# Weights of the second feed-forward quad split up and moved into the attention stage of a fused attention and two-MLP kernel

## The reference, cut to what matters

```python
# attention: batch 4, heads 8, seq 576, head_dim 64; factor 4
out_d = sm_attn(q_d, k_d, v_d)             # q, k, v averaged over groups of 4 tokens
mask = np.abs(pos[:, None] - pos[None, :]) < factor
scores = np.where(mask, scale * np.matmul(q, k.transpose(0, 1, 3, 2)), -1e9)
out_local = softmax(scores) @ v            # banded attention
x = np.repeat(out_d, factor, axis=2) + out_local      # -> 2304 tokens x 512
h = x @ w_in;  x = (h - np.tanh(h)) @ w_out                           # d_ff 2048
x = (1 / (1 + np.exp(-(x @ w_gate))) * (x @ w_val)) @ w_out           # d_ff 1536
```

## Time and profile before

| | |
|---|---|
| median of 3 runs | 947.53 us (947.15 to 951.25) |
| the profiled execution | 949.2 us, of it a span of 947.1 us from the first to the last instruction |
| granted TensorE clock, mean over the span | 0.971 |
| busy | PE 901.8 us (95%), DVE 577.1, ACT 387.3, POOL 300.5 |
| attention, up to the first product of quad 0 | 0 to 121.4 us |
| from there to where PE has no more gaps for a while | 121.4 to 165 us |

### The profile page before, as it was taken

One profiled execution on the slowest core, in us unless ns is written; L12 is line 12 of the kernel. 1 busy time (PEld: TensorE's weight loads), 2 busy tenths in 40 slices (PEclk: granted clock), 3 DMA queues, 4 the chain that ended last, 5 costly groups with the idle time before them and its releaser, 6 DMA issues.

```text
span 947.1 us, 15642 instructions
## 1 busy us (share of the span) xinstructions
PE 901.8 (95%) x6056; PEld 844.4 (89%) x6056; DVE 577.1 (61%) x901; ACT 387.3 (41%) x750; POOL 300.5 (32%) x251
## 2 busy tenths in 40 slices
PE   7877787999999999999998999999999999999997
PEld 5766577989999999999998999999999999999996
DVE  8777745666876566866668555556544456544445
ACT  4765645443533234433334544444322234222221
POOL 5978677674102000111015555741200001000000
PEclk8898969999999999999999999999999999999999
DMA  9677628667746464645421567679775555575411
GB/s 259 170 217 218 168 77 306 222 237 261 275 153 227 147 228 151 221 158 211 165 92 45 217 262 279 274 292 365 282 285 208 217 214 214 212 279 201 199 45 67
DMA packets 46089, 197.01 MB, mean 208 GB/s; under 512 B 3936, under 2 KB 15552, under 8 KB 33216
## 3 DMA queue, kind: packets, MB, share of 16 engines
q1 hardware_dynamic: 41984, 166.66, 48.9%
q0 software_dynamic: 4032, 29.36, 8.3%
HBM read 139.90 MB, written 56.10 MB: 207 GB/s over the span
## 4 chain that ended last, share of the span: by engine, by line
PE 79%; POOL 9%; DVE 3%; DMA 3%; issue 3%; ACT 2%; SPq 0%; POOLq 0%; DVEq 0%; ACTq 0%
PE banks L787 43%; PE banks L855 18%; PE banks L971 16%; DMA v_four<-in_v_dram 2%; POOL v_four L554 1%; POOL win L595 1%; POOL prob L561 1%; POOL mid L601 1%; POOL v_down L558 1%; ACT win L1035 1%; PE banks L765 1%; DMA qk<-in_k_dram 1%; POOL prob_d L561 1%; DVE x_op L1297 1%; PE banks L742 0%
## 5 line engine op out<-in xcount | busy, mean ns | idle before, releaser
L787 PE MATMUL banks<-x_op,pair 128*128 128x384 f32 x1512 | 278.5, 336 | 1.7 <-DVE cg_sum L1457 1.7
L787 PEld LDWEIGHTS banks<-x_op,pair 128*128 128x128 f32 x1512 | 266.7, 189 | 9.7 <-DVE cg_sum L1457 2.1
L855 PE MATMUL banks<-g_parts,mid 128*128 128x384 f32 x1152 | 228.4, 337 | 7.3 <-DVE x_all L1377 5.3
L855 PEld LDWEIGHTS banks<-g_parts,mid 128*128 128x128 f32 x1152 | 203.0, 189 | 10.2 <-DVE x_all L1377 7.3
L787 PE MATMUL banks<-x_op,win 128*128 128x384 f32 x1008 | 206.7, 342 | 4.3 <-ACT c_sum L1071 4.3
L787 PEld LDWEIGHTS banks<-x_op,win 128*128 128x128 f32 x1008 | 182.3, 193 | 5.5 <-ACT c_sum L1071 3.8
L971 PE MATMUL banks<-wout,p_parts 128*128 128x512 f32 x648 | 163.6, 393 | 1.7 <-issue 1.7
L1377 DVE TENSOR_TENSOR x_all<-banks,x_all 128x384 f32<-128x384 f32 x168 | 93.0, 555 | 83.3 <-PE banks L855 82.9
L971 PEld LDWEIGHTS banks<-wout,p_parts 128*128 128x128 f32 x648 | 120.3, 188 | 22.6 <-issue 2.1
L1482 DVE TENSOR_TENSOR x_all<-banks,x_all 128x512 f32<-128x512 f32 x90 | 62.1, 690 | 113.4 <-PE banks L971 113.4
L617 POOL DMA_DIRECT2D wout<-kept_out x12 | 6.4, 537 | 211.4 <-PE banks L971 211.4
(11 more groups left out here) (93 smaller groups left out, 1008.8 us busy)
## 6 DMA issues: line engine op xcount, KB each, us to landing
pair<-kept_pair SPq DMA_DIRECT2D x24, 1792.0 KB, 10.8
win<-kept_in SPq DMA_DIRECT2D x16, 1792.0 KB, 7.4
kept_pair<-pair SPq DMA_DIRECT2D x12, 1792.0 KB, 11.8
mid<-kept_mid POOLq DMA_DIRECT2D x16, 1024.0 KB, 5.1
kept_in<-win SPq DMA_DIRECT2D x7, 1792.0 KB, 6.8
wout<-kept_out POOLq DMA_DIRECT2D x12, 1024.0 KB, 11.7
kept_mid<-mid SPq DMA_DIRECT2D x7, 1024.0 KB, 7.0
kept_out<-wout SPq DMA_DIRECT2D x6, 1024.0 KB, 14.6
```

The source lines that it names most:

```text
L787: mm = pe.matmul(bk[:, 0:T], weights[:, w, p - 1, kk, :], x_op[:, p - 1, x, kk, :], start=(first and kk == 0 and a == 0), stop=(last and k ...
L855: mm = pe.matmul(bk[:, 0:T], w[:, wp, f, m * P:(m + 1) * P], g[:, gp, 2 * f + t, :], start=(f == 0 and a == 0), stop=(f == 1 and a == 2))
```

## The change

- GpSimd's round: `value_sums` comes last, behind `denominators` and `normalise`.
- `weight_sums(0)` is cut in two halves of two sums (rounds 2 and 3); `weight_high(0)` in two halves (ACT rounds 3 and 4); `weight_low(0)` in four quarters (GpSimd rounds 5 to 8). `plain_low(0)` is in round 9, `x_sums(0)` one sum each in rounds 11, 12, 13.
- Quad 1: `weight_sums(1)` in two halves in rounds 6 and 7, `weight_high(1)` in two halves in ACT's rounds 7 and 8, the low part on DVE (`second_weight_low`) ahead of its `first_quad(0)`, with a semaphore of its own.
- PE: product 5 of quad 0 ahead of the values of unit 15. ACT: the copy of C21 in round 16; `x_high(0, 4)` and `x_high(0, 3)` behind the copies of unit 15.
- SP: raw w_in of quad 1 in round 4 rather than 12, the stores of quad 0's weights two rounds later, raw w_mid of quad 1 right behind the last loads of v; for that the tiles of attention were laid out anew, so that w_mid's second slot is read by nobody once the scores are done.

```diff
@@ layout
-        low, high = Room(MID + MID_BYTES, CSUM), Room(CSUM + 2 * GS + 2 * 4 * T, limit - base)
+        low, high = Room(MID + 2 * MID_BYTES, CSUM), Room(CSUM + 2 * GS + 2 * 4 * T, limit - base)
+        scores = Room(MID + MID_BYTES, MID + 2 * MID_BYTES)
...
@@ SP
             def load_raw_mid(n):
+                if n == 1:
+                    sp.wait_ge(s_sl, UNITS)
+                    sp.wait_ge(s_sd, UNITS)
...
-                if u == 1:
+                if u == 2:
                     load_raw_mid(0)
-                if 6 <= u < 10:
-                    keep_early(kept_in[0], flat_f32(win[0][:, :, :, :, :]), s_wlo, 1, u - 6)
...
-                if u == 12:
+                if u == 4:
                     load_raw(1)
+                if 8 <= u < 12:
+                    keep_early(kept_in[0], flat_f32(win[0][:, :, :, :, :]), s_wlo, lows(0), u - 8)
...
+            load_raw_mid(1)
@@ GpSimd
+            def first_weight_low(piece):
+                dst, raw = unit_slot(0)
+                part = slice(piece * WS // 4, (piece + 1) * WS // 4)
+                pool.wait_ge(s_whi, highs(0))
...
-            for t in range(UNITS + 1):
-                if t > 0:
-                    value_sums(t - 1)
-                    denominators(t - 1)
-                    normalise(t - 1)
+            for t in range(1, UNITS + 1):
+                denominators(t - 1)
+                normalise(t - 1)
+                value_sums(t - 1)
                 if t == 2:
-                    weight_sums(0)
-                if t == 4:
-                    weight_low(0)
-                if t == 5:
+                    weight_sums(0, (0, 1))
+                if t == 3:
+                    weight_sums(0, (2, 3))
+                if 5 <= t < 9:
+                    first_weight_low(t - 5)
+                if t == 6:
+                    weight_sums(1, (0, 1))
+                if t == 7:
+                    weight_sums(1, (2, 3))
+                if t == 9:
                     plain_low(0)
-                if t == 10:
-                    x_sums(0)
-                if t == UNITS:
-                    x_last_sum(0)
-            weight_sums(1)
-            weight_low(1)
+                if 11 <= t < 14:
+                    x_sums(0, (t - 11,))
+            x_last_sum(0)
             weight_sums(2)
             weight_low(2)
@@ TensorE
+                if t == UNITS + 1:
+                    first_product(0, 5)
                 if t >= 2:
                     local_values(t - 2)
...
-                if t == UNITS + 1:
-                    first_product(0, 5)
@@ ScalarE
+            def half_weight_high(su, half):
+                dst, raw = unit_slot(su)
+                part = slice(half * WS // 2, (half + 1) * WS // 2)
+                act.wait_ge(s_wst, 4 * (su + 1))
...
-                if t == 3:
-                    weight_high(0)
+                if 3 <= t < 5:
+                    half_weight_high(0, t - 3)
+                if 7 <= t < 9:
+                    half_weight_high(1, t - 7)
+                if t == 6:
                     plain_high(0)
...
                 if t == UNITS:
                     copy_c(0, C22)
+                    copy_c(0, C21)
+                if t == UNITS + 1:
                     x_high(0, 4)
                     x_high(0, 3)
-                    weight_high(1)
-            first_quad(0, skip=2)
+            first_quad(0, skip=3)
@@ VectorE
             x_low(0, 4)
             write_x(UNITS - 1)
             x_low(0, 3)
+            second_weight_low()
```

More of the change, by code:

```diff
@@ L169, in attention_and_mlps @@
         PROBS = 2 * SLOTS * KW
-        qk = [high.tile(f"qk{i}", [P, 2, S]) for i in range(3)]
-        prob = []
-        qk_down = high.tile("qk_down", [P, 2, SD])
+        assert (UNITS - 1) % 3 == 0
+        qk = [room.tile(f"qk{i}", [P, 2, S]) for i, room in enumerate((scores, high, high))]
+        qk_down = scores.tile("qk_down", [P, 2, SD])
+        mask_b = scores.tile("mask_b", [P, SLOTS, KW], BF16)
+        ident_b = scores.tile("ident_b", [P, P], BF16)
+        band = scores.tile("band", [P, 140], BF16)
+        zeros_b = scores.tile("zeros_b", [P, 512], BF16)
         x_down = high.tile("x_down", [P, SD])
-        band = high.tile("band", [P, 140], BF16)
-        mask_b = high.tile("mask_b", [P, SLOTS, KW], BF16)
+        prob = [high.tile(f"prob{i}", [P, PROBS + 4]) for i in range(3)]
         v_win = [low.tile(f"v_win{i}", [KW, NW, P]) for i in range(2)]
@@ L246, in attention_and_mlps @@
         s_vlo = sem("val_low")
+        s_wlo1 = sem("second_weight_low")
         s_mhi = sem("plain_high")
@@ L617, in load_wout, with x_sums @@
                 pool.dma_start(flat_f32(wout[m % 2][:, :, :, :]), kept_out[m % Q2]).then_inc(s_wout[m % 2], 16)
[L619 removed]
+            def x_sums(s, steps=(0, 1, 2)):
                 at_s = s % NS
[L622 to L630, removed]
[L631 to L636 removed]
+                b11, b12, b22 = (x_block(at_s, *i) for i in ((0, 0), (0, 1), (1, 1)))
+                for step in steps:
+                    if step == 0:
+                        if s < NS:
+                            pool.wait_ge(s_x, PAIRS * -(-SUPER * (s + 1) // S))
+                        else:
+                            pool.wait_ge(s_bev, BLOCKS * Q1 * (at_s + 1))
+                        if s > 0:
+                            pool.wait_ge(s_xhi, 7 * s)
+                            pool.wait_ge(s_xlo, 7 * s)
+                        pool.tensor_tensor(tmp[:, 0, :, :], b22, b12, ALU.subtract).then_inc(s_t, 1)
+                    elif step == 1:
+                        pool.wait_ge(s_t, 4 * s + 1)
+                        pool.tensor_tensor(b12, b12, b11, ALU.subtract).then_inc(s_t, 1)
+                    else:
+                        pool.wait_ge(s_t, 4 * s + 2)
+                        pool.tensor_tensor(tmp[:, 1, :, :], b22, b12, ALU.subtract).then_inc(s_t, 1)
             def x_last_sum(s):
@@ L1036, in weight_high @@
                                ACT.Copy).then_inc(s_whi, 1)
+            def half_weight_high(su, half):
+                dst, raw = unit_slot(su)
+                part = slice(half * WS // 2, (half + 1) * WS // 2)
+                act.wait_ge(s_wst, 4 * (su + 1))
+                act.activation(dst[:, 0, :, :, :].rearrange("p o k n -> p (o k n)")[:, part], raw[:, :, :].rearrange("p o n -> p (o n)")[:, part],
+                               ACT.Copy).then_inc(s_whi, 1)
             def plain_high(pu):
@@ L1113, in first_quad @@
                     x_high(s - 1, 3)
-                copy_c(n, C21)
+                if skip < 3:
+                    copy_c(n, C21)
                 if last:
@@ L1412, in first_quad, with second_weight_low @@
                     x_low(s, 2)
+            def second_weight_low():
+                dst, raw = unit_slot(1)
+                dve.wait_ge(s_whi, highs(1))
+                dve.tensor_tensor(dst[:, 1, :, :, :].rearrange("p o k n -> p (o k n)"), raw[:, :, :].rearrange("p o n -> p (o n)"),
+                                  dst[:, 0, :, :, :].rearrange("p o k n -> p (o k n)").bitcast(F32), ALU.subtract).then_inc(s_wlo1, 1)
             x_low(0, 4)
```

61 lines of the change are left out of this document (34 added, 27 removed).

## The result

The changed kernel took 959.75 us (median of 4 runs, 956.83 to 960.59) against 947.34 us of the kernel before on the same chip (4 runs, 946.43 to 951.25): a ratio of 1.0098, 95% interval 1.007 to 1.0127. Timed again on another chip, in 12 runs, it took 956.23 us, ratio 1.0065 (1.0042 to 1.0088). So it is slower, by 0.65 to 1%. The forecast was 947.6 us with 0.67 for "within 0.5%", and its range ended at 953.0.

The account below looks back on a forecast made before the run. GpSimd and v_four's refill DMA were taken to bound attention. From 949.2 profiled, +0.2 attention, +0.8 loads of v, -0.9 behind attention gave 949.3, or 947.6 us as median; range 942.5 to 953.0, with 0.67 for within 0.5%.

Parts of the forecast that it names:

- Loads of v: SP's loads of v windows, behind v_four's refill, land later; cost 0.8 us (0 to 1.6), in unit 14.
- no gain in the ring: Attention's loop of waits among GpSimd, DVE, PE and v_four's DMA: putting value sums last gains nothing, lagging one unit more.
- shifts within its slack: Attention: outside unit 14, later loads of v cost little; extra work covers them or PE has room to shift.
- set-backs of 4.5 and 5.7 us: Attention rounds 3 and 7: delay of ACT and PE when ACT's half copies wait for GpSimd's weight sums.
- GpSimd's stream: Attention: GpSimd's work changes by +1.6 us in all, while its waits for v_four fall by 5.7 us.
- ACT's two blocks: Attention rounds 3 and 7: ACT's half copies wait for weight sums, costing 4.3 us (0.9 to 10.2).
- Handoff: Behind the attention: gaps of PE shrink but partly reappear; gain taken as 0.9 us (0.4 to 2.0).
- Rival one: Attention and behind it: stalls go as the change intends, clock stays up, ACT's 4.55 goes; 939.8 us, chance 0.18.
- Rival two: Attention rounds 3 and 7: ACT's waits pass on in full (10.2), v loads cost 1.6; 954.3 us, chance 0.15.
- Rival three: Quad 2's sums meet second_weight_low: DVE and GpSimd slow each other, tanh 2.0 us later; 949.6 us, chance 0.07.
- Signs: Trace marks for the forecast; right: quad 0 within 2 us of 121.4; wrong: before 118 or after 125.

Follow-up runs that it names:

- C: The kernel before with one edit, GpSimd's value sums moved behind denominators and scaling: 959.88 us, ratio 1.0087.
- A: The changed kernel with the value sums first in each unit again, everything else kept: 948.44 us, ratio 0.9985 to the kernel before.
- K: The changed kernel with ACT's half weight copies one round later (4, 5, 8, 9), run beside the changed kernel on one chip: 952.93 us, ratio 1.0033.
- L: A with ACT's half weight copies one round later: 947.75 us, ratio 0.9979 to the kernel before.
- B: The changed kernel with SP loading the windows of v for unit u+1 ahead of v_four's load for u+1: 956.94 us, ratio 1.0067 to the kernel before.
- F: B with ACT's half weight copies one round later (4, 5, 8, 9): 947.78 us, ratio 0.9988 to the kernel before.
- G: A with quad 2's weight copy ahead of quad 0's tanh on ACT and VectorE's second low part in round 10: 944.29 us, ratio 0.995.
- D: B with weight_high(2) moved ahead of quad 0's tanh in ACT's list: 956.65 us, ratio 1.0059 to the kernel before.
- H: G with ACT's half weight copies one round later and VectorE's low part in round 11: 942.69 us, ratio 0.9945 to the kernel before.
- M: H with GpSimd's three x steps in rounds 10 to 12 instead of 11 to 13: 942.16 us, ratio 0.9934 to the kernel before.

## Why the prediction was wrong

The step that failed is "Loads of v", and with it the sentence on `value_sums` last: "no gain in the ring. [...] It lags one unit more, no more". The term was 0.8 us (0 to 1.6), in one unit. The same order alone cost 0.87% in C, some 8 us. PE waited for these loads 13.1 us in five units there, and 12.0 us in five units in the changed kernel. The structure was seen: the prediction put these loads behind the refill in SP's order and counted 2.6 us for their issue, which the chain confirms (2.7). Two of its inputs were wrong:
- The landing. I took 3.66 to 5.8 us from other tiles' rows; the chain has 7.35, 8.64, 5.47, 5.51 and 5.09 us. The two longest are issued behind a raw weight tile. (In C the chain has 6.86, 4.70, 6.39 and 6.65; the first is behind a raw weight tile, the last two behind a store of weights.) That gives 10.0 and 11.3 us after the sums, where I had 6.3 to 8.4.
- The slack. I counted that PE "shifts within its slack" outside unit 14. It did not: five units were late. In the changed kernel one could blame the quicker ring, since PE's waits for GpSimd's probabilities fell from 13.7 us to 0.9. But in C they are still 10.4, and five units are late all the same. So the slack wasn't there in the kernel before either; what the quicker ring adds isn't shown.

The sentence fails in a second place. With the value sums last, their two steps (2.0 us) stand ahead of the weight sums, and ACT's waits grow by them. My set-backs of 4.5 and 5.7 us hold these 2.0 us, but I did not see that the order puts them there: in A, with the sums first, ACT waits 1.77 and 3.76 us.

Step by step:
- **GpSimd's stream, +1.6 - 5.7**: waits for `v_four` were to fall by 5.7 us, and this came: from 9.5 us in nine rounds to 3.6 in five. (The 4.7 at the start, outside the term, gave way to 8.3 us for the row sums.) With the sums first (A) 1.4 us are left beside the start's 4.4, less 8.1. But quad 0 began at 123.53 there, 2.15 later than before: what GpSimd no longer waited for, it waited for elsewhere, for VectorE's inverses 15.7 us where it had been 10.4. The term took it that a wait taken from GpSimd shortens the attention by as much; in A it did not.
- **ACT's two blocks, 4.3 (0.9 to 10.2)**: the mechanism is there, its price hangs on what else is late. In the changed kernel ACT waited 1.1 us in all in one execution and 2.5 in the other, instead of the 4 to 6 each that I named. Some 3 us were to be had by moving the copies (K), 0.0006 of the time with the sums first (L), and some 7.5 us with v first (B against F), between my 4.3 and its upper end. The sum of one number for each edit could not hold this: 1.0065 with both waits, 1.0067 without v_win's, 1.0033 without ACT's, 0.9988 without either.
- **Handoff, -0.9 (-0.4 to -2.0)**: -3.11 and +2.90 in the second and third stretch, -0.2 us; in A 28.94 and 60.80, which is -2.05 and +1.33, -0.7 us. Both parts come for the reasons named: the low part takes its 2.02 ahead of the first addition and PE's gap is back behind it (3.14), and the gap behind ACT shrank by 1.8 where I had up to 1.7. ACT's wait at quad 3 was to be 3 to 5 us; it was 6.12, for GpSimd can begin the sums only behind `weight_high(2)`.
- **Rival one** did not come: `weight_high(2)` is what GpSimd waits for, as said against it. What it described was reached only by moving that copy and VectorE's low part (G).
- **Rival two** had the side and nearly the time (954.3 us), but that is luck for the most part: it has 10.2 us from ACT's waits, of which K got back some 3, and 1.6 from the loads, which decide here.
- **Rival three** did not come in the changed kernel (2.02 us), for the reason given: GpSimd had ended and was waiting. D brought it about: 5.79 us. The page of the Trainium skill that I weighed (SBUF — State Buffer, section "SBUF: two separate sides") says that such instructions of VectorE and GpSimd lock each other out whole; D agrees: 3.91 and 1.88 us, one behind the other. I had its price as "up to twice 2.01"; in D it is 3.77 us on top, the rest of the other engine's instruction.
- **Signs**: I named quad 0 after 125 us as the mark of a wrong forecast; it came at 130.03 and 125.43. Of the marks of a right one, the wait for `v_four` came (in the rounds) and PE's gap ahead of product 3; ACT's two waits of 4 to 6 us, quad 0 within 2 us of 121.4 and 3 to 5 us at quad 3's sums did not.

## What to carry to other kernels

When a step is moved later on one engine, list every DMA that stands behind the wait that it feeds, in the issuing queue's order, and time the last of them from its own issue to its own landing; where the trace doesn't show that landing, a bound from another tile can be too low (5.8 us taken, 8.64 met). Don't grant the consumer a slack that no row shows: work it out unit by unit. Look also at what stands behind the moved step on its own engine. And two waits in one loop are tested together: taking away one alone can show nothing (B), while taking away both removes the loss (F).

## What the runs showed of the hardware

- The five loads of windows of v (512-byte rows) that the chain of the changed kernel passes landed 5.09 to 8.64 us after the issue of their last piece, while q and k of 288 KB had a median of 4.4 and 5.5 us in the same kernel. The five are late ones, since the chain picks what is waited for.
- In D and in H a two-input step on VectorE that met one on GpSimd ended only 1.88 us behind the end of GpSimd's. In H both paid, VectorE's low part (2.02 alone) and GpSimd's `v_four` sum (1.26 alone):
```profile
81.84 4.29 DVE L1355 TENSOR_TENSOR win<-win_raw,win 128x1792 fp32r<-128x1792 f32 x1
...
82.44 1.81 POOL L665 TENSOR_TENSOR x_tmp<-x_all 128x768 f32<-128x768 f32 x1
...
84.33 2.92 POOL L572 TENSOR_TENSOR v_four<-v_four 72x512 f32<-72x512 f32 x1
```
  GpSimd's step ends at 84.25, the low part 1.88 us after that, at 86.13, and the `v_four` sum 1.12 us after that. The low part began at 81.84, while GpSimd's scaling still ran (to 82.48), so it sat through the rest of that one and the whole next one. The time doesn't show it: G, with the low part a round earlier (2.52 us there) and the half copies not moved, took 1.6 us more.
- In the changed kernel a split of x took 3.23 us on VectorE (0.96 alone) beside the end of GpSimd's value sums and its x step, and PE's wait behind it was 4.58 us, against 2.28 before:
```profile
107.29 3.23 DVE L1349 TENSOR_TENSOR x_op<-x_tmp,x_op 128x768 fp32r<-128x768 f32 x1
107.91 1.79 POOL L671 TENSOR_TENSOR x_tmp<-x_all 128x768 f32<-128x768 f32 x1
...
112.12 1.98 PE L802 MATMUL banks<-prob_tl,v_win 70*64 70x64 f32 x32 [4.58 <-DVE x_all L1340]
```
  M moved the x steps, and the time didn't change by what can be told.
- Executions of one kernel differ by some 8 us in this program (944.56 to 952.99 us in 25 runs of the kernel before), and in the changed kernel's two profiles all of the difference lay in the attention.
